# Matmuls that nobody reads, put into three pauses of TensorE in the first step of an attention and two-MLP kernel

## What is computed

```python
def _attn_ref(r, k, v, w, u):
    for t in range(S):
        kt, vt, rt, wt = (k[:, :, t], v[:, :, t], r[:, :, t], w[:, :, t])
        cur = np.einsum('bhd,bhe->bhde', u[None] * kt, vt)
        y[:, :, t] = np.einsum('bhd,bhde->bhe', rt, state + cur)
        state = wt[:, :, :, None] * state + np.einsum('bhd,bhe->bhde', kt, vt)
    return y

def _moe_ref(x, w_in, w_out):       # x: 3072 x 384, w_in: 384 x 2048, w_out: 2048 x 384
    h = x @ w_in
    g = np.where(h > 0.0, h, np.exp(np.minimum(h, 0.0)) - 1.0)
    return g @ w_out

def _moe2_ref(x, w_in, w_out):
    h = x @ w_in
    return (h * (1.0 / (1.0 + np.exp(-1.702 * h)))) @ w_out
```

## Time and profile before

| | us |
|---|---|
| median of 3 runs | 979.79 (979.12 to 980.59) |
| profiled execution, its own time | 984.85 |
| its span in the trace | 983.0 |
| PE busy, share of the span | 943.9 (96%) |
| DVE, ACT, POOL busy | 550.1, 456.7, 93.7 |
| mean granted TensorE clock | 0.977 of full |

### The profile page before, as it was taken

The page is one execution under the profiler, slowest core; times in us unless marked ns, Lnnn a source line. Parts: engine busy times, 40 slices in busy tenths (PEclk is TensorE's granted clock), DMA queues, the critical chain, the costliest instruction groups (busy, mean ns, idle before and its releaser), DMA issues.

```text
span 983.0 us, 27123 instructions
## 1 busy us (share of the span) xinstructions
PE 943.9 (96%) x11872; PEld 918.3 (93%) x11872; DVE 550.1 (56%) x908; ACT 456.7 (46%) x874; POOL 93.7 (10%) x109
## 2 busy tenths in 40 slices
PE   3689899999899999999999999999999999999998
PEld 3589899999899999999999999999999999999998
DVE  8888576686585775866853444443434443434333
ACT  2546645547446456365464764333333333333332
POOL 1099200000000000000000641000000000000000
PEclk8589899999999999999999999999999999999999
DMA  6453211211301402112004620000000000000000
GB/s 184 97 146 91 56 51 26 56 51 27 94 15 28 102 20 63 51 26 56 28 2 158 231 68 1 25 1 24 0 24 0 22 2 6 18 1 25 1 25 25
DMA packets 15798, 47.30 MB, mean 48 GB/s; under 512 B 2864, under 2 KB 6832, under 8 KB 15696
## 3 DMA queue, kind: packets, MB, share of 16 engines
q1 hardware_dynamic: 13680, 40.85, 14.8%
q0 software_dynamic: 1536, 4.50, 1.7%
q10 hardware_dynamic: 480, 0.40, 0.2%
HBM read 35.71 MB, written 8.85 MB: 45 GB/s over the span
## 4 chain that ended last, share of the span: by engine, by line
PE 89%; POOL 4%; issue 2%; DVE 2%; DMA 1%; ACT 1%; DVEq 0%; SPq 0%; POOLq 0%
PE psum L1269 40%; PE psum L1282 40%; POOL w_split L382 4%; PE psum L1039 3%; PE psum L1153 1%; PE psum L1001 1%; PE psum L1145 1%; PE psum L1117 1%; PE psum L1082 1%; DMA staging<-weights_dram 1%; ACT blocks L441 1%; PE psum L1075 0%; DVE arena L701 0%; DMA arena<-r_channels_dram 0%; DVE blocks L755 0%
## 5 line engine op out<-in xcount | busy, mean ns | idle before, releaser
L1269 PE MATMUL psum<-x_hi,w_split 128*128 128x384 f32 x1536 | 395.9, 338 | 2.2 <-issue 2.1
L1282 PE MATMUL psum<-g_hi,w_split 128*128 128x384 f32 x1536 | 392.6, 337 | 0.0
L1269 PEld LDWEIGHTS psum<-x_hi,w_split 128*128 128x128 f32 x1536 | 281.4, 189 | 3.6 <-issue 3.6
L1282 PEld LDWEIGHTS psum<-g_hi,w_split 128*128 128x128 f32 x1536 | 278.3, 189 | 0.0
L1269 PE MATMUL psum<-x_lo,w_split 128*128 128x384 f32 x768 | 264.0, 344 | 4.8 <-DVE x_lo L792 3.2
L1282 PE MATMUL psum<-g_lo,w_split 128*128 128x384 f32 x768 | 262.0, 341 | 0.0
L816 DVE TENSOR_TENSOR g_lo<-gate,g_hi 128x384 fp32r<-128x384 f32 x256 | 149.5, 584 | 118.3 <-ACT g_hi L500 118.3
L500 ACT ACTIVATE g_hi<-gate 128x384 fp32r<-128x384 f32 x256 | 134.5, 525 | 170.9 <-DVE gate L811 88.2
L809 DVE TENSOR_TENSOR gate<-expo,psum 128x384 f32<-128x384 f32 x128 | 70.9, 554 | 162.6 <-ACT expo L496 162.6
L1269 PEld LDWEIGHTS psum<-x_lo,w_split 128*128 128x128 f32 x768 | 144.8, 189 | 6.8 <-issue 5.8
L1282 PEld LDWEIGHTS psum<-g_lo,w_split 128*128 128x128 f32 x768 | 144.8, 189 | 2.7 <-issue 0.3
(11 more groups left out here) (92 smaller groups left out, 479.0 us busy)
## 6 DMA issues: line engine op xcount, KB each, us to landing
v_sb<-v_tokens_dram SPq DMA_DIRECT2D x8, 576.0 KB, 5.8
arena<-w_channels_dram SPq DMA_DIRECT2D x14, 288.0 KB, 4.8
arena<-k_channels_dram SPq DMA_DIRECT2D x14, 288.0 KB, 4.8
arena<-r_channels_dram SPq DMA_DIRECT2D x14, 288.0 KB, 4.5
x_scratch<-x_sb SPq DMA_DIRECT2D x7, 576.0 KB, 3.3
arena<-x_scratch SPq DMA_DIRECT2D x1, 4032.0 KB, 12.5
staging<-weights_dram SPq DMA_DIRECT2D x9, 384.0 KB, 3.6
blocks<-weights_dram SPq DMA_DIRECT2D x9, 384.0 KB, 3.6
```

Of the source, the lines that this page charges most:

```text
L1269: mm = pe.matmul(hidden(f), w_tile(f, lo, m * P), xx, start=n == 0, stop=n == 3 * KT - 1)
L1282: mm = pe.matmul(acc(to, m), w_tile(f, lo, (KT + m) * P), gg, start=f == 0 and n == 0, stop=f == NF - 1 and n == 2)
```

## The change

A helper issues `count` matmuls of 384 columns, with a 128x128 tile of `w_split` as weights and the first 384 columns of `w_split` as the moving operand. It is called three times: 2 matmuls ahead of `keys_values(0, 0)`, 9 behind it, and 16 behind `first_outputs()`. Two waits stand ahead of the first call: that the first block of `w_split` is written, and that ACT has read bank 7. Nothing else is changed, and no engine but PE has a new instruction.

```diff
+                def keep_busy(bank, count):
+
+                    for _ in range(count):
+                        pe.matmul(bank[:, 0:T], w_tile(0, 0, 0), w_split[:, 0:T], start=True, stop=True)
+
...
                 first_turn(0)
                 first_turn(1)
+                pe.wait_ge(whi_done, 1)
+                pe.wait_ge(off_done, N_OFF)
+                keep_busy(FIRST[7], 2)
                 keys_values(0, 0)
+                keep_busy(FIRST[7], 9)
                 first_outputs()
+                keep_busy(FIRST[1], 16)
                 up(0, 0, 0)
                 near(1)
```

## The result

The changed kernel took 987.22 us (median of 4 runs, 984.89 to 991.51) against 980.19 for the kernel before (4 runs, 979.12 to 982.14): a ratio of 1.0057, interval 1.0035 to 1.0079. It is slower by 0.6%, where 1.2 us faster was forecast.

A forecast was written before the change was run, and what follows sets the result against it. PE, busy 96% of the span, was taken as the bound, with POOL's chain hiding part of its gains. Earlier outputs (0.6) and last load (0.6) made 1.2 us off 979.79, so 978.6, range 976.2 to 981.0.

The forecast's parts named there:

- The added matmuls: PE's first-step pauses: the first two hidden, at most 0.1 us late; nine and sixteen cost nothing at full clock.
- The first paragraph: Whole span: PE busy 96%, so ending the first step earlier ends the kernel equally earlier at most, later PE work untouched.
- The clock: PE's granted clock: at the full level from somewhere between 38 and 43 us until past 100.
- The outputs and `x_lo`: `first_outputs` in step 0: an earlier clock rise gains 0.6 us, bounds 0.77 gained and 0.69 lost; `x_lo` at about 48.9.
- PE 2.8 earlier from 55 on: After the first MLP products: 2.2 plus 0.6 us gained on PE, hidden by POOL; pause ahead of 108.08 becomes about 4.1.
- The last load: Weight load of block 15: shares less with k of the next step, 0.6 us gained, bounds 0 and 3.2.
- The clock falls further on: Rival, chance 0.12: longer pause ahead of step 1's `outputs` drops the clock, price 3.0 us, giving 982.2.
- It doesn't do what it says: Rival, chance 0.10: fillers run at half clock, clock rises no sooner, `first_outputs` 0.69 us late, giving 980.5.

The follow-up runs named there:

- e9: Changed kernel plus 50 small matmuls (shift 255), SP's load of r for step 1 also waiting for ACT's two transfers: 981.61 us, ratio 1.0001 to the kernel before.
- e1: Changed kernel with its 27 added matmuls cut to 32 columns of weights and moving operand: 984.04 us against 981.74 for the kernel before, ratio 1.0029.
- e11: Kernel before plus 60 small matmuls in the third pause, a shift of 240 instructions: 978.68 us, ratio 0.9973 to the kernel before.
- e8: Kernel before plus 48 small matmuls in the third pause, a shift of 192 instructions: 985.76 us, ratio 1.0037 to the kernel before.
- e7: Kernel before plus 32 small matmuls in the third pause, a shift of 128 instructions: 984.90 us, ratio 1.0041 to the kernel before.
- e5: Changed kernel plus 50 small matmuls behind the sixteen, a shift of 255 instructions: 981.27 us against 981.16 for the kernel before, ratio 1.0001.

## Why the prediction was wrong

**The step that failed** is the first of the sum, "The added matmuls". It priced them by their durations in pauses (0.64, 1.59, 2.83) and took them as free where the pause covered them. The first paragraph rests on the same thing, "since PE's later work is untouched". What they cost isn't duration. They are 55 instructions ahead of all later code, and this moves the places where PE stands still for code. Put at nothing, this term measured 5.9 us: the same 27 matmuls take 987.22 at a shift of 55 and 981.27 at 255 (by the ratios to the kernel before, 1.0057 and 1.0001, it is 5.5). The code waits up to 510 us fell by 5.8 between these two (14.7 and 8.9), in one profile of each. The row that could have warned me was in the trace: PE stopping for 1.8 us, named issue, between two matmuls of one accumulation, where no semaphore stands.

**The clock** did as forecast: full from 36.2, a little sooner than the "38 to 43" given, through the first product of the MLP. It didn't last until 100: it fell at 56.7, behind the standstill of 2.55, and was back at 60.1.

**The outputs and `x_lo`**, 0.6 forecast: the copies L960 came earlier as worked out, at 45.58 in an execution that was already 1.03 late at 30.15 against the earlier trace rows's 29.12 for the same work, so 0.97 gained. But `x_lo` was ready 9.95 us after the scores began (50.43 - 40.48), against 10.10 in the earlier trace rows: 0.15 gained. I had not followed SP: the earlier end of the outputs frees the load of r, and e9 shows that this holds the small transfers up.

**PE 2.8 earlier from 55 on** failed. Ahead of the outputs of step 1 it waited 2.67, not 4.1: the two standstills took 4.4, where the kernel before had lost 1.8 at its one.

```profile
110.32 1.99 PE L1150 MATMUL psum<-blocks,v_sb 64*48 64x64 f32 x96 [2.67 <-DVE state L780]
```

They start at 110.32, 2.24 later than the earlier trace rows; 1.03 of this was there before the first added instruction, and 1.2 arose behind it.

**The last load**, 0.6 forecast: nothing. It took 6.84, and POOL's chain, which I took to depend on POOL alone, was by then held by ACT (the chain of the changed kernel, 71 to 102 us):

```profile
71.49 0.53 ACT g_hi L500
72.02 0.74 ACT w_split L516
72.76 0.07 issue
72.84 4.69 POOL w_split L382 x4
...
94.64 6.84 DMA staging<-weights_dram
101.48 0.02 issue
101.50 0.02 ACT w_split L516
```

POOL stood still for 2.01 us ahead of 72.84 until ACT had rounded the block. ACT does so behind `g_hi`, which waits for DVE's `gate`, and DVE came to it late: its L695 had begun at 64.59, when PE's first level of step 1 was done behind the standstill of 1.89, against 62.48 in the kernel before.

**The rivals.** None of them had this cause. "The clock falls further on" got the sign with another mechanism, and its place didn't show it: the pause there was as long as before. "It doesn't do what it says" was wrong in its premise.

**What is open.** What sets the length of a standstill at a place of the code is only partly settled: 0.2 to 2.9 us were seen, and up to 2.9 and down to 1.9 at the same place (2497 records in, in e1 and in the changed kernel). Behind 537 us, where PE has wide matmuls alone, no trace has one over 0.15. Nor is it settled why 240 beats 0 and 256 by 3 us when its waits aren't shorter in the profile.

The Trainium skill ("Runtime: NRT & Kernel Launch", section "Instruction fetch mechanics") says that an engine's code comes in blocks of 16 KiB, 256 instructions, the next one being fetched while one runs, and that the cost of crossing a boundary is mostly hidden. The block agrees: packets of 16 KB, standstills 256 apart, and the time of before back at 255 and 256. Most crossings are hidden here too, but not the ten of the changed kernel that cost 14.7 us, 2.55 and 1.89 at two in a row. If all were hidden, this term would be nothing, as the prediction had it.

## What to carry to other kernels

In a kernel that keeps one engine busy over long straight code, an edit anywhere in that engine's program moves all code behind it, and here that alone was worth from 3 us less (e11) to almost 5 us more (e8) of 981. Before a small gain or loss is put down to what an edit does, time the edit once with its instruction count brought back to the same place by harmless instructions (here 256 in all), and time the count alone. In the profile, number the engine's instructions: idle times named `issue` that stand at one and the same count within a block of 256, each behind a packet of a queue named `instruction`, are waits for code. And when a stage is made faster, follow every queue that its end releases: here the load of r took back what the outputs had gained.

## What the runs showed of the hardware

- TensorE stood still at places a multiple of 256 instructions apart, for up to 2.55 us in the changed kernel and 2.91 in e1, and 181 of 182 such standstills over 0.2 us ended 1.05 to 1.62 us after a 16 KB packet of the queue `instruction`.
- In the changed kernel both of step 1 fell among small matmuls, which use up code fast: from 41 to 42 us, at full clock, 76 matmul records went by, each with a weight load. At that rate 256 instructions last 1.7 us, an estimate; the packet of 53.72 and the time behind it took 2.4.
- Behind the loop's jump back TensorE stood still once in each of the 17 traces, 35 records on, for 0.25 us (e7) to 1.53 (e11), and started again 1.54 to 1.76 us after such a packet. The view of the changed kernel names DVE as the releaser there, so the cause of these isn't settled.
- A semaphore increment at the head of TensorE's program is not free: 200 of them put the first matmul at 31.76 us, and in the trace one starts every 0.15, where 100 records of small matmuls in e5 took 3.35.
- A standstill of 2.55 us between dense stretches was followed by the lower clock level from 56.7 to 60.1.
- The slower of ACT's two transfers of 24 KB landed after 2.6 us in e9, where SP held the load of r (288 KB a piece) back for it, and after 4.0 in e5, where that load was issued within the 1.5 us in which ACT issued its two.
